# Attention, gated mixer and channel MLP on one core: a four-step head with paired score tiles and a separate gate buffer

## The reference

```python
def _attn_ref(q, k, v):                    # 4 batches, 8 heads, 576 rows, head dimension 64
    scores = scale * np.matmul(q, k.transpose(0, 1, 3, 2))
    mask = block_i >= block_j              # blocks of 64 positions
    scores = np.where(mask, scores, -1000000000.0)
    attn = np.exp(scores - np.max(scores, axis=-1, keepdims=True))
    attn = attn / (np.sum(attn, axis=-1, keepdims=True) + 1e-09)
    return np.matmul(attn, v)
def _moe_ref(x, w_in, w_spatial, b_spatial, w_out):      # the mixer
    h = np.maximum(x @ w_in, 0.0); u, v = h[..., :d_ff // 2], h[..., d_ff // 2:]
    v_n = (v - mean(v)) / np.sqrt(var(v) + 1e-06)
    v_s = np.einsum('ts,bsd->btd', w_spatial, v_n) + b_spatial[None, :, None]
    return (u * v_s) @ w_out
def _moe2_ref(x, g_ln, w_ch1, w_ch2):                     # the channel MLP
    xn = (x - mean(x)) / np.sqrt(var(x) + 1e-06) * g_ln
    return x + np.maximum(xn @ w_ch1, 0.0) @ w_ch2
```

## Time and profile before

| | |
|---|---|
| median of 3 runs | 891.14 us (890.93 to 891.88) |
| the profiled execution | 891.44 us, its span 889.3 us |
| mean granted TensorE clock | 0.994 |
| TensorE busy | 862.5 us (97% of the span) |
| DVE, ACT, POOL busy | 360.0, 282.7, 201.5 us |
| chain that ended last | PE 90%, issue 4%, POOL 2%, ACT 2%, DVE 1% |

### The profile page before, as it was taken

One profiled execution on the slowest core, in us unless ns is written; L12 is line 12 of the kernel. 1 busy time (PEld: TensorE's weight loads), 2 busy tenths in 40 slices (PEclk: granted clock), 3 DMA queues, 4 the chain that ended last, 5 costly groups with the idle time before them and its releaser, 6 DMA issues.

```text
span 889.3 us, 13334 instructions
## 1 busy us (share of the span) xinstructions
PE 862.5 (97%) x5000; PEld 704.6 (79%) x5000; DVE 360.0 (40%) x806; ACT 282.7 (32%) x752; POOL 201.5 (23%) x289
## 2 busy tenths in 40 slices
PE   6999999999999999999889999999999999999998
PEld 3556778667787677876878999999999999999997
DVE  4677734357443574434575322132122122132111
ACT  4566543444534445334335211111111111111110
POOL 3565544514334153331272000000000000000000
PEclk9999999999999999999999999999999999999999
DMA  5443121221212302004325002002001101100100
GB/s 181 129 146 128 52 86 44 90 94 32 68 41 91 98 27 67 14 25 156 110 95 175 33 1 107 1 1 87 19 0 59 47 0 38 68 0 35 36 1 36
DMA packets 37680, 56.02 MB, mean 63 GB/s; under 512 B 2749, under 2 KB 20157, under 8 KB 37630
## 3 DMA queue, kind: packets, MB, share of 16 engines
q1 hardware_dynamic: 37630, 55.34, 18.8%
HBM read 45.90 MB, written 9.44 MB: 62 GB/s over the span
## 4 chain that ended last, share of the span: by engine, by line
PE 90%; issue 4%; POOL 2%; ACT 2%; DVE 1%; DMA 0%; ACTq 0%; POOLq 0%; DVEq 0%
PE psum L962 23%; PE psum L964 22%; PE psum L963 22%; PE psum L925 7%; PE psum L939 6%; PE psum L954 3%; PE psum L957 3%; PE psum L920 2%; ACT probs L531 1%; PE psum L1036 1%; POOL rstd L458 0%; DMA qk_raw<-qk 0%; PE psum L928 0%; POOL unit_raw L497 0%; POOL x_r L466 0%
## 5 line engine op out<-in xcount | busy, mean ns | idle before, releaser
L884 DVE SCALAR_TENSOR_TENSOR h_r<-psum,h_r 128x384 fp32r<-128x384 f32 x96 | 53.5, 557 | 287.4 <-ACT h_r L676 287.4
L676 ACT ACTIVATE h_r<-psum 128x384 fp32r<-128x384 f32 x96 | 47.2, 492 | 340.5 <-PE psum L964 340.5
L962 PE MATMUL psum<-xn_r,units_r 128*128 128x384 f32 x384 | 129.6, 337 | 0.0
L964 PE MATMUL psum<-xn_r,units_r 128*128 128x384 f32 x384 | 129.4, 337 | 0.0
L963 PE MATMUL psum<-xn_r,units_r 128*128 128x384 f32 x384 | 128.9, 336 | 0.0
L714 DVE TENSOR_REDUCE neg_max<-psum 128x1 f32<-128x128 f32 (+4 forms) x160 | 82.9, 539 | 76.8 <-PE psum L928 49.2
L964 PE MATMUL psum<-units_r,h_r 128*128 128x512 f32 x288 | 113.7, 395 | 0.0
L963 PE MATMUL psum<-units_r,h_r 128*128 128x512 f32 x288 | 113.5, 394 | 0.0
L962 PE MATMUL psum<-units_r,h_r 128*128 128x512 f32 x288 | 111.9, 389 | 0.0
L531 ACT ACTIVATE probs<-psum,neg_max 128x128 f32<-128x128 f32 (+4 forms) x160 | 89.9, 566 | 66.6 <-DVE neg_max L714 66.0
L447 POOL TENSOR_SCALAR probs<-probs,row_inv 128x128 f32<-128x128 f32 (+4 forms) x160 | 89.9, 581 | 74.1 <-DVE row_inv L727 74.1
(11 more groups left out here) (95 smaller groups left out, 1482.2 us busy)
## 6 DMA issues: line engine op xcount, KB each, us to landing
qk_raw<-qk SPq DMA_DIRECT2D x32, 576.0 KB, 4.0
unit_raw<-w_ch SPq DMA_DIRECT2D x32, 256.0 KB, 3.1
y_norm<-y_scratch SPq DMA_DIRECT2D x6, 768.0 KB, 5.7
y_res<-y_scratch SPq DMA_DIRECT2D x6, 768.0 KB, 4.6
out<-y_res SPq DMA_DIRECT2D x18, 256.0 KB, 2.1
v_raw<-vN SPq DMA_DIRECT2D x16, 256.0 KB, 2.9
y_scratch<-mix_buf SPq DMA_DIRECT2D x16, 256.0 KB, 2.0
w_raw<-w_in SPq DMA_DIRECT2D x8, 256.0 KB, 5.0
```

What stands on the lines that cost most here:

```text
L676: act.activation(h_hi[:, f % HR, :], h_bank[:, f % 2, 0:CHUNK], ACT.Relu).then_inc(h_hi_done, 1)
L884: dve.scalar_tensor_tensor(h_lo[:, f % HR, :], h_bank[:, f % 2, 0:CHUNK], 0.0, h_hi[:, f % HR, :].bitcast(F32), ALU.max, ALU.subtract).the ...
L962: pe.matmul(dst, a_hi, b_hi, start=start, stop=False)
L964: return pe.matmul(dst, a_lo, b_hi, start=False, stop=stop)
```

## The change

A head has four steps. Step 0 has the value product of head n-1 first, then the scores of tiles 3, 2 and 0 of head n+1 (score_first: tile 3 on partitions 0 to 63, tiles 2 and 0 on 64 to 127, the masks behind), then the transposes of tiles 3, 0 and 2 of head n. Step 1 has nothing of attention on TensorE. Step 2 has the scores of tiles 4 and 1 (score_second, each as two halves on the two sets of partitions) and the transposes of tiles 1 and 4. In the value product the order of left and right parts is another. Each head has one mixer group at each of steps 0, 2 and 3, and in the fourth and eighth head of a batch also at step 1.

The processed order of tiles is 3, 0, 2, 1, 4 (TILES). Tiles 0 and 2 share a PSUM bank, for scores and again when transposed; ACT waits with the exponentials of a pair for both maxima (PEAKS) and with the copies for both transposes (MADE). ACT copies tiles 0, 2, 4, and DVE 3 and 1. From head 8 on the second scores use a bank of the first ones, and wait for their exponentials. The gate halves of batches 0 to 2 go into a buffer of their own (gate_r, through gated(b)) instead of x_r, so split_x of the next batch waits only for the u groups; it is spread over heads (x_split_at) instead of coming in one block, and piece k = 3 comes in step 1 of the next batch's first head. POOL normalises the first three tiles one step block earlier (step 1 of the head before). The weight pieces are spread otherwise, POOL splits a piece one head after ACT, and SP issues its load one head later. The value-product and score semaphores count two and four a head.

```diff
-        s_bank = psum[:, 0:3, :]
-        t_bank = psum[:, 3:5, :]
+        m_bank = psum[:, 3:5, :]
         o_bank = psum[:, 5, :]
-        m_bank = psum[:, 6:8, :]
+        t_bank = psum[:, 6:8, :]
         acc_bank = psum[:, 0:3, :]
-        h_bank = psum[:, 3:5, :]
-        xt_bank = psum[:, 5:8, :]
+        h_bank = psum[:, 6:8, :]
+        xt_bank = psum[:, 3:6, :]
         ...
-        STEPS = 5
-        DVE_TILES, ACT_TILES = [0, 1, 3], [2, 4]
+        STEPS = 4
+        DVE_TILES, ACT_TILES = [3, 1], [0, 2, 4]
         SPLIT_Q = 392
         ...
-        GROUP_STEPS = [[2, 3], [0, 1, 2, 3], [0, 1, 2, 3], [0, 1, 2], [0, 1, 2, 3], [0, 1, 2, 3], [1, 2], [0, 1, 3]]
-        assert sum(len(r) for r in GROUP_STEPS) == GROUPS and len(GROUP_STEPS) == H and STEPS - 1 not in sum(GROUP_STEPS, [])
+        def t_place(t):
+            return (0, 0) if t in (3, 1) else (1, KEYS[2] if t == 0 else 0)
+        def transposed_free(pe, n, t):
+            if t == 3 and n >= 1:
+                pe.wait_ge(t_copied_dve, len(DVE_TILES) * n)
+            elif t == 0 and n >= 1:
+                pe.wait_ge(t_copied_act, len(ACT_TILES) * n)
+            elif t == 1:
+                pe.wait_ge(t_copied_dve, len(DVE_TILES) * n + 1)
+            elif t == 4:
+                pe.wait_ge(t_copied_act, len(ACT_TILES) * n + 2)
+        TILES = [3, 0, 2, 1, 4]
+        PEAKS = {3: 1, 0: 3, 2: 3, 1: 5, 4: 5}
+        AT = [TILES.index(t) for t in range(NT)]
+        MADE = {3: 1, 0: 3, 2: 3, 1: 4, 4: 5}
+        FIRST = 3
+        def second_banks(n):
+            return psum[:, 2:4, :] if n < H else psum[:, 1:3, :]
+        def score_of(n, t):
+            if t == 0:
+                return psum[:, 1, KEYS[2]:KEYS[2] + KEYS[0]]
+            if t == 2:
+                return psum[:, 1, 0:KEYS[2]]
+            if t == 3:
+                return psum[:, 0, 0:KEYS[3]]
+            if t == 1:
+                return second_banks(n)[:, :, HALF:HALF + P]
+            return second_banks(n)[0:LAST, :, 0:HALF]
+        GROUP_STEPS = [[0, 2, 3], [0, 2, 3], [0, 2, 3], [0, 1, 2, 3], [0, 2, 3], [0, 2, 3], [0, 2, 3], [0, 1, 2, 3]]
+        assert sum(len(r) for r in GROUP_STEPS) == GROUPS and len(GROUP_STEPS) == H
             ...
-            return [] if step == 0 else (late(n, 1, 3) if step == 1 else []) + late(n, step, 2)
+            return late(n, step, 2)
+        def x_split_at(n, step):
+            b, h = n // H, n % H
+            if step == 1:
+                return [(b - 1, KD - 1)] if h == 0 and b >= 1 else []
+            return [(b, h // 2 - 1)] if b == 0 and h in (2, 4, 6) else [(b, h - 4)] if b and 4 <= h <= 6 else []
         ...
-        PIECES_PER_HEAD = [1] * H + [1, 1, 1, 2, 2, 2]
+        PIECES_PER_HEAD = [2] + [1] * (H - 2) + [0, 2, 2, 1, 2, 2]
             ...
+            for t in TILES[:FIRST]:
+                normalise(0, t)
             for n in range(HEADS):
                 for step in range(STEPS):
                     if step == 0:
-                        for t in range(3):
-                            normalise(n, t)
-                    elif step == 1:
-                        for t in range(3, NT):
+                        for t in TILES[FIRST:]:
                             normalise(n, t)
                         if n + 2 < HEADS:
                             scale_q(n + 2)
-                    if 3 <= step and step - 3 < len(pieces_at(n)):
-                        split_piece(pieces_at(n)[step - 3])
+                    elif step == 1 and n + 1 < HEADS:
+                        for t in TILES[:FIRST]:
+                            normalise(n + 1, t)
+                        for i in pieces_at(n - 1):
+                            split_piece(i)
                 ...
-                act.wait_ge(maxed, NT * n + t + 1)
+                act.wait_ge(maxed, NT * n + PEAKS[t])
                     ...
-                    act.wait_ge(grouped, GROUPS * b)
+                    act.wait_ge(grouped, GROUPS * (b - 1) + S0)
                 ...
                         if n >= 1:
                             output_right(n - 1)
-                        if n and n % H == 0:
-                            for k in range(KD):
-                                split_x(n // H - 1, k)
+                        if n + 1 < HEADS:
+                            for t in TILES[:FIRST]:
+                                exp_tile(n + 1, t)
+                        copy_transposed(n, 0)
+                        copy_transposed(n, 2)
+                    elif step == 1:
+                        for b, k in x_split_at(n, 1):
+                            split_x(b, k)
                     elif step == 2:
-                        copy_transposed(n, 2)
+                        copy_transposed(n, 4)
                         if n + 1 < HEADS:
-                            exp_tile(n + 1, 3)
-                    elif step == 3:
-                        if n + 1 < HEADS:
-                            exp_tile(n + 1, 4)
+                            for t in TILES[FIRST:]:
+                                exp_tile(n + 1, t)
                     else:
-                        copy_transposed(n, 4)
-                    if step == 2:
-                        piece(n, 0)
-                    if step == 4:
-                        piece(n, 1)
+                        for b, k in x_split_at(n, 3):
+                            split_x(b, k)
+                        for i in pieces_at(n):
+                            split_piece(i)
                 ...
                     if step == 0:
-                        if n + 1 < HEADS:
-                            for t in range(3):
-                                max_tile(n + 1, t)
-                    elif step == 1:
                         if n >= 1:
                             output_left(n - 1)
-                        copy_transposed(n, 0)
-                        copy_transposed(n, 1)
-                        if n and n % H == 0:
-                            for k in range(KD):
-                                split_x(n // H - 1, k)
+                        if n + 1 < HEADS:
+                            for t in TILES[:FIRST]:
+                                max_tile(n + 1, t)
+                        invert(n, 1)
+                        copy_transposed(n, 3)
+                    elif step == 1:
+                        if n + 1 < HEADS:
+                            invert(n + 1, 0)
+                        for b, k in x_split_at(n - 1, 3) + x_split_at(n, 1):
+                            split_x(b, k)
                     elif step == 2:
                         if n + 1 < HEADS:
-                            max_tile(n + 1, 3)
-                            invert(n + 1, 0)
-                    elif step == 3:
-                        if n + 1 < HEADS:
-                            max_tile(n + 1, 4)
-                        copy_transposed(n, 3)
-                    else:
-                        if n + 1 < HEADS:
-                            invert(n + 1, 1)
+                            for t in TILES[FIRST:]:
+                                max_tile(n + 1, t)
+                        copy_transposed(n, 1)
             ...
+            def score(n, dst, half, rows, keys):
+                return pe.matmul(dst, qk_raw[half, n % QS, 0, rows], qk_raw[half, n % QS, 1, keys],
+                                 start=True, stop=True)
+            def mask(dst, half):
+                return pe.matmul(dst, row_pick[half, :], row_mask[half, :], start=False, stop=True,
+                                 skip_group_check=True)
+            LOW, HIGH = slice(0, BLOCK), slice(BLOCK, P)
+            def rows_of(t):
+                return slice(P * t, P * t + ROWS[t])
+            def score_first(n):
+                pe.wait_ge(q_scaled, n + 1)
+                if 1 <= n <= H:
+                    pe.wait_ge(exped, NT * (n - 1) + FIRST)
+                elif n > H:
+                    pe.wait_ge(exped, NT * n)
+                score(n, score_of(n, 3), LOW, rows_of(3), slice(0, KEYS[3]))
+                score(n, score_of(n, 2), HIGH, rows_of(2), slice(0, KEYS[2]))
+                mask(score_of(n, 2)[:, KEYS[2] - BLOCK:KEYS[2]], HIGH)
+                score(n, score_of(n, 0), HIGH, rows_of(0), slice(0, KEYS[0]))
+                mask(score_of(n, 0)[:, KEYS[0] - BLOCK:KEYS[0]], HIGH).then_inc(scored, 1)
+                mask(score_of(n, 3)[:, KEYS[3] - BLOCK:KEYS[3]], LOW).then_inc(scored, 1)
+            def score_second(n):
+                if n >= H:
+                    pe.wait_ge(exped, NT * n + FIRST)
+                elif n >= 1:
+                    pe.wait_ge(exped, NT * n)
+                for half, part in enumerate((LOW, HIGH)):
+                    score(n, score_of(n, 4)[:, half, :], part, rows_of(4), slice(HALF * half, HALF * (half + 1)))
+                for half, part in enumerate((LOW, HIGH)):
+                    last = score(n, score_of(n, 1)[:, half, :], part, rows_of(1), slice(P * half, P * (half + 1)))
```

(35 more changed lines are left out.)

142 lines of the change are left out of this document (56 added, 86 removed).

## The result

The changed kernel takes 902.13 us (median of four, 899.61 to 904.38) against 891.3 us for the kernel before on the same chip: ratio 1.012, 95% interval 1.0093 to 1.0148. It is slower by 11 us, where 882.7 with a range of 873 to 894 had been predicted. The profiled execution took 902.4 us, 900.6 of it span.

The account below looks back on a forecast made before the run. TensorE, busy 97% of the span, bounds the kernel. Mixer heads go from 336.84 to 327.4 us (-9.4), attention-only heads +2.0, tail -1.0: span 889.3 to 880.9, time 882.7 us, range 873 to 894.

Parts of the forecast that it names:

- The granted clock: Mixer heads: clock falls to half after the wait before each batch's first output group, 1.6 us each, 4.8 us more.
- VectorE's split of x: Attention-only heads 3, 5, 7: a DVE split (0.75 us) in front of the maxima adds 0.65 us each.
- ScalarE's splits of weights: Mixer heads: piece loads and ACT's third copy called covered, ACT 152.99 busy of 336.84 us; no wait listed for weight splits.
- The pieces: Mixer heads: scores -14.0, value product -4.5, transposes +8.4, group seams -5.7 us, giving 308.1 us before new waits.
- The second scores: Step 2: tile 4 at 0.63 us plus tile 1 in halves at 0.46 with a drain, 0.36 without.
- First output group: Behind the last spatial group: waits 1.95 us for the gate, three times, 5.9 us.
- Second group of head 3: Step 1: waits 1.1 us for a bank ACT reads late; with 0.2 in head 7, 4.0 us in all.
- First value group: Step 0 of a batch's first head: last quarter waits 1.5 us for the x split, three times, 4.6 us.
- after idle of this size the clock fell: First output groups: idle of 1.81 us was followed by clock 0.50 for 3.41 us, so 1.6 us more each.
- The prediction's +2: Attention-only heads: loop of 7.1 us against 7.20, plus 0.65 in heads 3, 5, 7; about +2 us, bounds -2 and +6.
- value product 1.55: Attention-only heads: the value product's 1.55 us counted as one term of the 7.1 us loop.
- rival 2: Attention-only heads lose the clock: 3.2 us more in each of seven heads, +22 us, 905 us in all; 11%.

Follow-up runs that it names:

- e10_all_bare: Kernel of e8_all without any idle matmul in heads 0 to 7; 868.49 us, ratio 0.9706 to 0.9773.
- e8_all: Changed kernel with x splits, gate splits, first output group, ScalarE's mixer reads and weight splits moved, ten idle matmuls in heads 0 to 7; 875.85 us.
- e9_all_short: Kernel of e8_all with three idle matmuls instead of ten in each of heads 0 to 7; 866.16 us.
- e11_waits_filled: Changed kernel with nine unread idle matmuls ahead of the first value group and the first output group of each batch; 896.08 us.
- e1_split_late: Changed kernel with VectorE's split in heads 3, 5, 7 (13 to 15 of later eights) moved behind its copy of tile 1; 891.47 us.
- e13_all_scores_first: Kernel of e10_all_bare with the order of e12_scores_first; 858.05 us, ratio 0.9621 to the kernel before.
- e12_scores_first: Changed kernel with next head's first scores before the last head's value product, maxima and exponentials before output copies; 873.78 us.
- e2_filler_heads: Changed kernel with unread matmuls before the value product in heads 0 to 7: three each, ten in heads 3, 5, 7; 896.93 us.

## Why the prediction was wrong

The steps that failed, by size. The granted clock was charged 4.8 us, behind the first output groups alone; it cost about 12.8 in the mixer heads and 4.6 in the attention-only heads. VectorE's split of x was charged 0.65 us in each of three attention-only heads and cost 1.77. ScalarE's splits of weights were called covered, and made a wait of 2.0 us. The pieces themselves were priced rightly.

**Point by point, profiled execution against profiled execution.** Predicted span 880.9, measured 900.6, so 19.7 us are missed: 16.0 in the mixer heads (343.4, predicted 327.4), 8.4 in the attention-only heads (+10.4, predicted +2), -4.0 at the start, -0.7 in the tail (-1.7, predicted -1.0).

**The pieces** were right to 0.02 us each, and their sum nearly: 308.1 predicted, and 312.2 measured (310.7 and the last value product) in e10_all_bare, of which about 2 are the waits that are left. With the kernel before against that, the change is worth 24.6 us in the mixer heads. Three right passes stand in one row from 217.83, ahead of left 0's second pass at 218.21; the rule on the Trainium skill's page "TensorE: Matmul & The Clock Gate" (Part 3), that matmuls start and end in program order, is contradicted here too. The second scores take 1.08, priced 1.09 with a drain between its two shapes and 0.99 without. The Trainium skill's page "TensorEngine Tiling (Array Packing)", Key Properties, says that a change of the tiling mode drains the array; the 1.08 agrees.

**The waits in the mixer heads** were found at their places, and nearly in size. First output group: 2.42, 2.42 and 2.00 us, predicted 1.95; ScalarE's split of x (289.61, 0.67 us) stood in front of its gate half. Second group of head 3: 1.05 (0.79, and 0.26 a step later), predicted 1.1. First value group: 2.24 (5.15 for 2.91 of work), predicted 1.5; the 0.7 is a mixer read on ScalarE ahead of the split (204.21 to 204.69) and slower small operations on VectorE. Not seen at all was the second scores' wait in batch 0:

```profile
118.79 0.74 PE L934 MATMUL psum<-qk_raw 64*64 64x288 f32 x2 [2.02 <-ACT probs L569]
```

ScalarE was splitting weights (112.87, 1.24 us) ahead of the read that VectorE's statistics and then its maxima waited for. The prediction had called these splits covered, from ScalarE's busy share. Placed at the end of their step, they leave half of it (0.92 in e8_all, 0.99 and 1.00 in e9_all_short and e10_all_bare). That step failed: I had priced the instruction and not its place.

**The clock** was the largest single term of the 16.0: 8.0, with 3.4 for this wait and three smaller ones of batch 0 and of the second scores (0.67, 0.35 twice), 2.1 for the first value groups, and the remaining 2.5 in the pieces' sum and the other waits. 4.8 us were predicted for the clock, as three stretches of 1.6 behind the first output groups. Measured against the same pieces at full clock, B lost about 12.8 us; it has 26.6 us at 0.50, and half of that would be 13.3. Behind the wait at 118.79:

```profile
118.84:122.25 3.41, 3.41 (x17) 1.80 (x18) 2.27 (x7) 1.62 (x6) 2.40 (x5) 0.50 0.00 0
```

and another 3.4 us like it behind that. The step "after idle of this size the clock fell" was applied to one of the kinds of wait only, not to the first value groups nor to the second scores. e11_waits_filled, which fills six of these waits and removes none, shows the effect, apart from the stretch behind its one unfilled wait. As a rule for each wait the step doesn't hold: five of seven lost the clock here, three of the same seven in e1_split_late. So the prediction's three stretches behind the three output groups (two here, none in e1_split_late) were part luck.

**The attention-only heads.** The 10.4 us are 5.3 for the split (three times 1.77), 4.6 for the clock (the heads of 8.84, 10.74 and 9.06 us against 7.43 or 9.19) and 0.5 for the loop. The prediction's +2 had 1.95 for the split and nothing for the clock. It summed the loop to 7.1 us against 7.20 before, and that sum was near (7.43; the copies, the small operations and hand-overs made 0.3). The clock had been ruled out because a wait of 0.51 us a head had kept it; three waits of 0.35, 0.32 and 0.96 did not. What I did not see at all is a chance missed and no part of the 10.4: this loop is closed only because the value product stands first. With the scores first a head takes 5.8 us, so against that order each of these heads gives away 1.5 us, and has the waits over which the clock falls. In the sum it appears as the line "value product 1.55", beside a first score of 1.33; I never asked whether either had to be in it. Of rival 2 the mechanism was right and the size was not: not seven heads at half clock for 22 us, but three stretches of 3.4 us at 1.6 each.

The DVE split was taken at 0.65 us for three heads, and cost 1.77. In the kernel before it took 0.75 us each time, and no row before showed it beside GpSimd. Moved away (e1_split_late) it cost nothing in the two such heads whose split lies in A.

**The start** gained 4.0 us that I had not looked at. Part of it may be chance: the value product of head 0 starts at 16.74 us here, and at 16.49 to 18.58 in the five kernels that change nothing before it. By the lengths of its pieces, TensorE ran at full speed earlier: second scores take 1.11 us at 13.39 in the changed kernel, nearly their later 1.08, while in the kernel before three transposes still take 0.83 at 17.08 and 0.48 at 25.37. The granted clock reads 1.00 in both and doesn't tell it; what sets it was not tried.

What stays open: why the median of e1_split_late moved by 10.7 us, of which A explains 6.0 in the profiled execution; its ten runs lie between 887.71 and 898.57, and the stretches at half clock fall differently in each. What picks the waits behind which the clock falls is open too. e13_all_scores_first still loses the clock in and right behind A, and has its split in the wrong place for its order; neither fillers nor the old place were tried with it.

## What to carry to other kernels

For each loop without cover, write down which pieces have to be in it, not only how long it is: a piece that could stand beside it, put at its head, costs its full length in every turn. A wait is read from the queue of the engine that ends it, instruction by instruction; a busy share of 40% says nothing of what stands in front. Price a wait on TensorE twice, once as idle and once as what may follow at half clock (1.6 us for 3.4 us at 0.50, behind three to five of seven waits here); and when work must be moved, move it within the queue that holds it up, since moving TensorE's groups only moved the waits.

## What the runs showed of the hardware

**VectorE and GpSimd hold each other up.** A subtraction of 128x576 in fp32 took 1.82 us on VectorE beginning beside a scaling on GpSimd, 1.98 us beside GpSimd's own subtraction, and 2.77 us in e13_all_scores_first. It took 0.74 us in e1_split_late in the middle of GpSimd's three normalises: there GpSimd paid, with 2.38 us for the three against 1.59 in e12_scores_first. Over the kernel GpSimd pays too: all its normalises take 100 us in the changed kernel and 93 in the one before, most of it in the form 128x128, 0.53 us each against 0.37:

```profile
L483 POOL TENSOR_SCALAR probs<-probs,row_inv 128x128 f32<-128x128 f32 x32 | 16.8, 526 | 0.0
```

The Trainium skill, page "Trainium Architecture — The Big Picture", section "What this means for kernel authors", says that within the engine side only the pair of ports which the two share contends, and that this is a lock and not a split of bandwidth. One pair of rows agrees in size: VectorE kept its 0.74 us, and GpSimd's three normalises grew by 0.79. Which of the two holds the ports at a given time no row shows.

**The granted clock fell over small waits, and not each time.** In attention-only heads with waits of 0.35, 0.32 and 0.96 us in 7.42 it fell to 0.50, the lower of its two levels (1.2 of 2.4 GHz), now and then; with the longest of the three filled (e2_filler_heads) it stayed up in A, and in the kernel before heads with a wait of 0.51 us had kept it. How often it falls differs even between kernels whose attention-only heads are the same: their mean granted clock in A lies between 0.88 and 0.91. Of longer waits the same holds: one of 2.0 us before the second scores was followed by 6.8 us at 0.50 in the changed kernel and by none in e1_split_late and e11_waits_filled, which leave it as it is.
